# Up projection on TensorE: the low parts of the last 64 inputs, for gate and value side by side on half of the rows each

## The chip, the core and the metric

The kernel runs on one core of a Trainium2 chip. A core has a matrix engine (TensorE, PE in the profile; its weight loads are a row of their own, PEld), a vector engine (VectorE, DVE), a scalar engine (ScalarE, ACT), a general engine (GpSimd, POOL) and a queue engine (SyncE, SP) that issues the DMAs here. The metric is the device time of one execution in microseconds (us).

## The reference

What is computed is an mLSTM recurrence over 16 heads of 768 steps and then two gated feed-forward layers on all 1536 tokens. The up projection, on which the change works, is `x @ w_gate` and `x @ w_val`:

```python
def _moe_ref(x, w_gate, w_val, w_out):       # x (1536, 320), w_gate and w_val (320, 1536), w_out (1536, 320)
    gate = 1.0 / (1.0 + np.exp(-(x @ w_gate)))
    val = x @ w_val
    return (gate * val @ w_out).astype(np.float32)

def _moe2_ref(x, w_gate, w_val, w_out, rms_g):
    rms = np.sqrt(np.mean(x * x, axis=-1, keepdims=True) + 1e-06)
    xn = x / rms * rms_g
    g = xn @ w_gate
    silu = g * (1.0 / (1.0 + np.exp(-g)))
    val = xn @ w_val
    return (silu * val @ w_out).astype(np.float32)
```

The output of the mLSTM goes through `_moe_ref` (layer 0 below) and then `_moe2_ref` (layer 1).

## The kernel before, in words

TensorE multiplies in a type of 32 bits that keeps fewer bits than float32 (F32R). To come close to float32, each operand is held as a high part and a low part (`x_hi`, `x_lo`; `wgv_hi`, `wgv_lo` for the weights of gate and value; `wo_hi`, `wo_lo` and `h_hi`, `h_lo` for the down projection), and a product is the sum of three: high by high, high by low, low by high.

The 320 inputs of a layer are cut into 128 + 128 + 64. The 64 of the last slot (index 2) stand twice, in rows 0 to 63 and in rows 64 to 127, of `x_hi` and `x_lo`; in the weights the upper 64 rows are replaced by the low part (`split_gv`, L375). So one pass over 128 rows gives high by high and low by high of these 64 at once.

`hidden` (L869) computes one tile of 128 of the 1536 hidden features, number f = 0 to 11, for gate (m = 0) and value (m = 1), each in its own PSUM bank. A product for gate is 8 passes, each of which is one weight load and one MATMUL instruction: three (L896, L897, L899) for each of the two full slots, two (L896, L897) for the last. Gate and value together are 16 passes. The banks alternate between two pairs (0 and 1, 2 and 3), so that tile f waits until VectorE has read the banks of tile f - 2 (`hf_done`).

Layer 0 has `NB0` = 6 blocks k of 256 tokens, layer 1 `NB1` = 4 blocks of 384 tokens; each block is 12 calls of `hidden`, and then `project` (L902), the down projection, 3 passes for each f and each 128 tokens (L914, L915, L916). In layer 0 the order in TensorE's program is written by hand: the table `WEAVE` says which pieces of the mLSTM follow after which slot. Piece S is the product of queries and keys (L803): 8 products for each of 12 tiles n, in pairs of heads, one on rows 0 to 39 and one on rows 64 to 103 of the array, each pair into two banks; the profile shows two MATMULs for each product. After S of an even n (slot 2 of a block, in the first block slot 3) `hidden` follows directly; after S of an odd n (slot 6, in the first block 7) the transposes of piece T (L761) come. Pieces N (L822, L830), K (L840) and D (L780, L782) use 120 or 128 rows.

The epilogue of a tile is: ScalarE sigmoid of the gate bank (L527), VectorE product with the value bank into `hf` (L717; in layer 1 also L715), ScalarE `h_hi` (L537), VectorE `h_lo` (L722). In layer 1 the results of `project` stand in banks 0, 1 and 2, which `hidden` uses too, so both functions wait for each other's readers (`hf_done`, `oe_done`).

Of the kernel before, what the change touches and what calls it, by code (L numbers as in the profile page):

```python
# [4 lines left out]
F32 = mybir.dt.float32  # L5
# [5 lines left out]
B, H, S, D = 2, 8, 768, 40  # L11
DM = H * D
FF = 1536
P = 128
NJ = S // P
NT = B * NJ
# [7 lines left out]
NF = FF // P  # L24
# [10 lines left out]
T1 = 3  # L35
# [40 lines left out]
def mlstm_moe_kernel(nc, gates, qk_t, q_t, vok, w_gv, w_o, rms_g, out):  # L76
    ctx = ExitStack()

    def sem(name):
        return ctx.enter_context(nc.semaphore(name))  # L80

    with ctx:
        def sb(name, shape, dt):
            return ctx.enter_context(nc.sbuf_tensor(name, shape, dt))
# [18 lines left out]
        x_hi = sb("x_hi", [P, NT, 3, P], F32R)  # L103
        x_lo = sb("x_lo", [P, NT, 3, P], F32R)
        h_hi = sb("h_hi", [P, NF * N1], F32R)
        h_lo = sb("h_lo", [P, NF * N1], F32R)
        wgv_hi = sb("wgv_hi", [P, GVC, 3, CW], F32R)
# [47 lines left out]
        bank = [ctx.enter_context(nc.psum_tensor(f"bank{i}", [P, 512], F32)) for i in range(8)]  # L155
# [18 lines left out]
        def raw_of(lay, c):  # L174
            ring = (raw0, raw1)[lay]
            r = ring[c % len(ring)]
            if c < GVC:
                return r.rearrange("p (k c) -> p k c", k=3)
            return r[:, 0:FC * DM].rearrange("p (k c) -> p k c", k=FC)
# [5 lines left out]
            return bank[2 * ((n // NF + f) % 2 if lay == 0 else f % 2) + 1]  # L185

        def o_bank(lay, m):
            return bank[2 * (m // B % 2) + m % B] if lay == 0 else bank[m]

        def y_slot(n):  # L190
            return 1 if n == 1 else 0
# [44 lines left out]
        hf_done = sem("hf_done")  # L236
# [5 lines left out]
        yo_done = sem("yo_done")  # L242
        oe_done = sem("oe_done")
        whi0 = sem("whi0")
        wlo0 = sem("wlo0")
        split0 = sem("split0")
        whi1 = sem("whi1")
        wlo1 = sem("wlo1")
        split1 = sem("split1")
# [95 lines left out]
        def _(pool):  # L345
# [22 lines left out]
            def split_gv(lay, c):  # L368
                whi, wlo, split = ((whi0, wlo0, split0), (whi1, wlo1, split1))[lay]
                r = raw_of(lay, c)  # L370
                pool.wait_ge(whi, c + 1)
                pool.tensor_tensor(wgv_lo[:, c, :, :], r[:, 0:2, :], wgv_hi[:, c, 0:2, :].bitcast(F32),  # L372
                                   ALU.subtract).then_inc(wlo, 1)
                pool.wait_ge(wlo, c + 1)
                pool.tensor_tensor(wgv_hi[64:P, c, 2, :], r[64:P, 2, :], wgv_hi[64:P, c, 2, :].bitcast(F32),  # L375
                                   ALU.subtract).then_inc(split, 1)
                pool.wait_ge(split, c + 1)

# [7 lines left out]
            def split(lay, c):  # L386
                if c < GVC:
                    split_gv(lay, c)
                else:
                    split_o(lay, c)  # L390
# [32 lines left out]
            for g in range(NG):  # L423
                nh = min(GH, H - GH * g)
                cs = slice(g * GH * D1, (g * GH + nh) * D1)
# [36 lines left out]
        def _(act):  # L462
# [76 lines left out]
            for k in range(NB0):  # L539
                for slot in range(NF + 4):  # L540
                    if slot < NF:
                        sigmoid(0, NF * k + slot, slot)
                        h_high(0, NF * k + slot, slot)
                    for what in WEAVE[k][slot]:
                        piece(what)
                    if k == 0:
                        for c in SPLIT_AT.get(slot, []):
                            high(0, c)
                    if k == NB0 - 1 and slot < NF and slot % FC == FC - 1:
                        high(1, 2 * (slot // FC))  # L550
                        high(1, 2 * (slot // FC) + 1)
                    if slot >= NF and slot % 2:
                        m = B * k + (slot - NF) // 2
                        act.wait_ge(o_done, m + 1)
                        if m >= B:
                            act.wait_ge(ot_done, m - B + 1)
                        act.activation(y_tok[:, 1 + m % B, 0:DM], o_bank(0, m)[:, 0:DM], ACT.Square,
                                       scale=float(DM) ** -0.5, accum_out=meansq_in[:, m % B:m % B + 1]).then_inc(ss_done, 1)
# [199 lines left out]
        def _(pe):  # L758
# [93 lines left out]
                        pe.wait_ge(r_exp, 2)  # L852
                    turn(bank[7], 1 + n % B).then_inc(ot_done, 1)

            def hidden(lay, k, f, halves=(0, 1)):
                c, i = f // FC, f % FC
                w = (N0, N1)[lay]
                n = NF * k + f if lay == 0 else F1 + NF * k + f
                if lay == 0:
                    if f == 0:  # L860
                        pe.wait_ge(x_done, B * k + B)
                        if k:
                            pe.wait_ge(hf_done, n)
                        else:

                            pe.wait_ge(x_done, B)
                    elif f == 1 and k:
                        pe.wait_ge(yo_done, B * k)
                    elif f >= 2:  # L869
                        pe.wait_ge(hf_done, n - 1)  # L870
                    if k == 0 and i == 0:
                        pe.wait_ge(split0, 2 * (c + 1))
                    xs = slice(B * k, B * k + B)
                else:
                    if f == 0 and 0 in halves:
                        pe.wait_ge(x2_done, T1 * (k + 1))
                        pe.wait_ge(hf_done, n)
                    if k == 0:
                        if f == 1:
                            pe.wait_ge(yo_done, NT)  # L880
                    elif f == 0:
                        pe.wait_ge(oe_done, T1 * (k - 1) + halves[-1] + 1)
                    elif f == 1 and 0 in halves:
                        pe.wait_ge(oe_done, T1 * k)
                    if f >= 2:
                        pe.wait_ge(hf_done, n - 1)
                    if k == 0 and i == 0:
                        pe.wait_ge(split1, 2 * (c + 1))
                    xs = slice(T1 * k, T1 * k + T1)
                cs = slice(i * P, (i + 1) * P)  # L890
                for m in halves:
                    ps, done = ((g_bank, g_done), (v_bank, v_done))[m]
                    ps = ps(lay, n, f)[:, 0:w]
                    wc = 2 * c + m
                    for s in range(3):
                        pe.matmul(ps, wgv_hi[:, wc, s, cs], x_hi[:, xs, s, :], start=(s == 0), stop=False)  # L896
                        mm = pe.matmul(ps, wgv_hi[:, wc, s, cs], x_lo[:, xs, s, :], start=False, stop=(s == 2))  # L897
                        if s < 2:
                            pe.matmul(ps, wgv_lo[:, wc, s, cs], x_hi[:, xs, s, :], start=False, stop=False)  # L899
                    mm.then_inc(done, 1)  # L900

            def project(lay, k, t, half):  # L902
                n0 = NF * k if lay == 0 else F1 + NF * k
                h = (h0, h1)[lay]
                if half == 0:
                    pe.wait_ge(hf_done, n0 + (NF - 1 if lay == 0 or t < 2 else NF))
                ts = slice(t * P, (t + 1) * P)
                ps = o_bank(lay, B * k + t if lay == 0 else t)[:, 0:DM]
                for f in range(half * NF // 2, (half + 1) * NF // 2):
                    if t == 0:  # L910
                        pe.wait_ge(h_done, n0 + f + 1)
                        if k == 0 and f % FC == 0:
                            pe.wait_ge((split0, split1)[lay], GVC + f // FC + 1)
                    pe.matmul(ps, h[0][:, f, ts], wo_hi[:, f, :], start=(f == 0), stop=False)  # L914
                    pe.matmul(ps, h[0][:, f, ts], wo_lo[:, f, :], start=False, stop=False)  # L915
                    mm = pe.matmul(ps, h[1][:, f, ts], wo_hi[:, f, :], start=False, stop=(f == NF - 1))  # L916
                if half == 1:
                    mm.then_inc(o_done, 1)
# [11 lines left out]
                        piece(what)  # L930
            for k in range(NB1):
                for f in range(NF):
                    if k and f == 0:
                        hidden(1, k, 0, (0,))
                        hidden(1, k, 0, (1,))
                    elif k and f == 1:
                        hidden(1, k, 1, (1,))
                        hidden(1, k, 1, (0,))
                    else:
                        hidden(1, k, f)  # L940
                    if k == 0 and f in (1, 3):
                        piece(("O", NT - B + f // 2))
                for t in range(T1):
                    for half in range(2):
                        project(1, k, t, half)
# [66 lines left out]
```

## Time and profile before

| | |
|---|---|
| time, median of 3 runs | 526.01 us (525.93 to 529.76) |
| the profiled execution: its own time | 525.22 us |
| its span in the trace | 523.5 us |
| PE busy | 483.7 us (92%), 3417 MATMULs in the trace |
| DVE, ACT, POOL busy | 250.0, 193.8, 123.2 us |
| up projection: L896, L897, L899 | 720 + 720 + 480 MATMULs |
| granted TensorE clock, mean of the span | 0.970 of full speed |

Times are us from the start of the span unless marked ns. A MATMUL's record begins when it begins to read and its length is modelled, so consecutive records overlap (0.28 us long, 0.12 us apart): the distance between starts is what a pass costs. In the groups of section 5 of the page and in the waits, the arrow names what an engine waited for.

### The profile page before, as it was taken

Reading aid. Unit: us, or ns where it says so; the run is one execution under the profiler, and the core shown is the slowest. Engines: PE = TensorE matmul, PEld = TensorE weight load, DVE = VectorE, ACT = ScalarE, POOL = GpSimd, SP = SyncE. Lnnn points to the kernel's source line nnn. Section 1 sums busy time; section 2 is a strip of 40 time slices with the busy share of each in tenths; the row PEclk is TensorE's granted clock in tenths of the full one; section 3 lists DMA queues with packets and bytes.
Section 4 is the critical chain, followed back from the end, with each engine's and each line's share of the span. In section 5 each row is a group of like instructions: output and inputs, shape, how many; then the busy total and the mean of one; then the engine's idle time right before and its main releaser. Section 6 shows DMA issues by size and latency. Waiting matters only on the chain.

```text
span 523.5 us, 8507 instructions
## 1 busy us (share of the span) xinstructions
PE 483.7 (92%) x3417; PEld 469.5 (90%) x3417; DVE 250.0 (48%) x517; ACT 193.8 (37%) x390; POOL 123.2 (24%) x125
## 2 busy tenths in 40 slices
PE   3659885989998999899899999999999999999997
PEld 2658884979997999899899989999999999999997
DVE  6664996165435724561561552762155135604540
ACT  4347532544265325524441574431133123303320
POOL 3749654211411411141001488500000000000000
PEclk9677987999999999999999999999999999999999
DMA  7435360021102201210112142000000000000001
GB/s 256 153 104 156 105 205 2 1 64 57 41 25 61 74 1 30 63 39 1 52 63 114 45 159 85 0 1 14 25 2 1 26 14 0 1 26 13 1 1 38
DMA packets 11148, 27.74 MB, mean 53 GB/s; under 512 B 1366, under 2 KB 5510, under 8 KB 11110
## 3 DMA queue, kind: packets, MB, share of 16 engines
q1 hardware_dynamic: 11110, 27.20, 16.1%
q8 instruction: 27, 0.44, 0.3%
q14 instruction: 11, 0.09, 0.1%
HBM read 25.23 MB, written 1.97 MB: 52 GB/s over the span
## 4 chain that ended last, share of the span: by engine, by line
PE 75%; DVE 11%; ACT 6%; issue 4%; POOL 3%; DVEq 0%; ACTq 0%; POOLq 0%
PE bank L896 16%; PE bank L897 16%; PE bank L899 10%; PE bank L914 8%; PE bank L916 8%; PE bank L915 8%; PE bank L830 3%; DVE hf L717 2%; DVE h_lo L722 1%; PE bank L822 1%; ACT tail L485 1%; ACT L485 1%; PE bank L803 1%; ACT L527 1%; POOL wgv_lo L372 1%
## 5 line engine op out<-in xcount | busy, mean ns | idle before, releaser
L896 PE MATMUL bank<-x_hi,wgv_hi 128*128 128x256 f32 (+1 forms) x720 | 221.0, 312 | 6.2 <-DVE hf L717 3.4
L897 PE MATMUL bank<-x_lo,wgv_hi 128*128 128x256 f32 (+1 forms) x720 | 217.0, 306 | 0.0
L899 PE MATMUL bank<-x_hi,wgv_lo 128*128 128x256 f32 (+1 forms) x480 | 147.2, 307 | 0.0
L896 PEld LDWEIGHTS bank<-x_hi,wgv_hi 128*128 128x128 f32 x720 | 138.9, 193 | 8.5 <-DVE hf L717 4.1
L897 PEld LDWEIGHTS bank<-x_lo,wgv_hi 128*128 128x128 f32 x720 | 139.0, 193 | 0.4
L537 ACT ACTIVATE h_hi<-hf 128x256 fp32r<-128x256 f32 (+1 forms) x120 | 55.3, 461 | 170.1 <-DVE hf L717 170.1
L914 PE MATMUL bank<-wo_hi,h_hi 128*128 128x320 f32 x288 | 90.5, 314 | 5.6 <-DVE h_lo L722 4.2
L899 PEld LDWEIGHTS bank<-x_hi,wgv_lo 128*128 128x128 f32 x480 | 92.6, 193 | 0.0
L915 PE MATMUL bank<-wo_lo,h_hi 128*128 128x320 f32 x288 | 89.9, 312 | 0.0
L916 PE MATMUL bank<-wo_hi,h_lo 128*128 128x320 f32 x288 | 89.9, 312 | 0.0
L717 DVE TENSOR_TENSOR hf<-sg,bank 128x256 f32<-128x256 f32 (+1 forms) x120 | 56.6, 472 | 68.5 <-ACT sg L527 45.7
L722 DVE TENSOR_TENSOR h_lo<-hf,h_hi 128x256 fp32r<-128x256 f32 (+1 forms) x120 | 76.2, 637 | 0.6
L715 DVE TENSOR_TENSOR sg<-sg,bank 128x384 f32<-128x384 f32 x48 | 26.6, 554 | 101.1 <-PE bank L897 91.5
L527 ACT ACTIVATE sg<-bank 128x256 f32<-128x256 f32 (+1 forms) x120 | 50.0, 417 | 38.5 <-PE bank L897 38.1
L914 PEld LDWEIGHTS bank<-wo_hi,h_hi 128*128 128x128 f32 x288 | 54.9, 191 | 6.5 <-DVE h_lo L722 4.4
L915 PEld LDWEIGHTS bank<-wo_lo,h_hi 128*128 128x128 f32 x288 | 54.9, 191 | 0.0
L916 PEld LDWEIGHTS bank<-wo_hi,h_lo 128*128 128x128 f32 x288 | 54.9, 191 | 0.0
L742 DVE SCALAR_TENSOR_TENSOR y_tok<-bank,rstd,g_row 128x320 f32<-128x320 f32 x12 | 6.6, 551 | 55.7 <-POOL rstd L443 55.7
L780 PE MATMUL bank<-causal,ident_b 128*128 128x512 bf16 x24 | 10.6, 442 | 19.2 <-DVE d_rhs L621 8.5
L571 ACT ACTIVATE y_tok<-bank 128x320 f32<-128x320 f32 x12 | 5.3, 438 | 52.8 <-PE bank L916 52.8
L780 PEld LDWEIGHTS bank<-causal,ident_b 128*128 128x128 bf16 x24 | 2.5, 105 | 24.6 <-issue 10.5
L830 PE MATMUL bank<-step,tail 128*128 128x41 f32 x192 | 23.2, 282 | 0.7 <-DVE tail L637 0.6
(106 smaller groups left out, 449.0 us busy)
## 6 DMA issues: line engine op xcount, KB each, us to landing
step<-in_w_gv SPq DMA_DIRECT2D x7, 576.0 KB, 3.9
step<-in_vok SPq DMA_DIRECT2D x12, 324.0 KB, 3.2
step<-in_qk_t SPq DMA_DIRECT2D x24, 160.0 KB
raw_x<-in_w_gv SPq DMA_DIRECT2D x5, 576.0 KB, 4.0
raw_p<-in_w_gv SPq DMA_DIRECT2D x4, 576.0 KB, 5.4
y<-y_tok SPq DMA_DIRECT2D x12, 160.0 KB, 1.8
step<-in_vok SPq DMA_DIRECT2D x10, 180.0 KB, 3.7
step<-in_q_t SPq DMA_DIRECT2D x10, 180.0 KB, 2.5
```

The lines of the kernel that those rows point to most:

```text
L527: act.activation(sg[:, f % 2, 0:w], g_bank(lay, n, f)[:, 0:w], ACT.Sigmoid).then_inc(sg_done, 1)
L537: act.activation(h[0][:, f, :], hf[:, f % 2, 0:w], ACT.Copy).then_inc(hhi_done, 1)
L715: dve.tensor_tensor(sg[:, u, 0:w], sg[:, u, 0:w], g_bank(lay, n, f)[:, 0:w], ALU.mult).then_inc(silu_done, 1)
L717: dve.tensor_tensor(hf[:, u, 0:w], sg[:, u, 0:w], v_bank(lay, n, f)[:, 0:w], ALU.mult).then_inc(hf_done, 1)
L722: dve.tensor_tensor(h[1][:, f, :], hf[:, f % 2, 0:w], h[0][:, f, :].bitcast(F32), ALU.subtract).then_inc(h_done, 1)
L830: mm = pe.matmul(bank[base(n) + 2][:, h * D1:(h + 1) * D1], wexp[b][:, i, c, :], va[b][:, h * D1:(h + 1) * D1], start=True, stop=True)
L896: pe.matmul(ps, wgv_hi[:, wc, s, cs], x_hi[:, xs, s, :], start=(s == 0), stop=False)
L897: mm = pe.matmul(ps, wgv_hi[:, wc, s, cs], x_lo[:, xs, s, :], start=False, stop=(s == 2))
L899: pe.matmul(ps, wgv_lo[:, wc, s, cs], x_hi[:, xs, s, :], start=False, stop=False)
L914: pe.matmul(ps, h[0][:, f, ts], wo_hi[:, f, :], start=(f == 0), stop=False)
L915: pe.matmul(ps, h[0][:, f, ts], wo_lo[:, f, :], start=False, stop=False)
L916: mm = pe.matmul(ps, h[1][:, f, ts], wo_hi[:, f, :], start=False, stop=(f == NF - 1))
```

## The change

In `hidden`, the two products of the last slot's low input part (`x_lo`, slot 2) now go over 64 rows only, where they take the high part of the weights alone: gate on rows 0 to 63, value on rows 64 to 127, one right behind the other, ahead of all other passes of the tile. The low by low term, which the 128-row pass held, is gone. For this the split of the weights is mirrored for value: chunk c odd keeps its high part in rows 64 to 127 and has the low part in rows 0 to 63. The other 14 passes stay as they were, in another order within a slot. So a tile has 16 MATMULs as before, 14 over 128 rows and 2 over 64.

In layer 1, `project` writes banks 4, 5 and 6 in place of 0, 1 and 2; `hidden` no longer waits for `oe_done`, `project` waits for it in place of `hf_done`, and the first two tiles of a block are no longer split or turned round.

```diff
         def o_bank(lay, m):
-            return bank[2 * (m // B % 2) + m % B] if lay == 0 else bank[m]
+            return bank[2 * (m // B % 2) + m % B] if lay == 0 else bank[4 + m]
...
-                pool.tensor_tensor(wgv_hi[64:P, c, 2, :], r[64:P, 2, :], wgv_hi[64:P, c, 2, :].bitcast(F32),
+                ls = slice(0, 64) if c % 2 else slice(64, P)
+                pool.tensor_tensor(wgv_hi[ls, c, 2, :], r[ls, 2, :], wgv_hi[ls, c, 2, :].bitcast(F32),
                                    ALU.subtract).then_inc(split, 1)
...
-            def hidden(lay, k, f, halves=(0, 1)):
+            def hidden(lay, k, f):
...
+                if f >= 2 or lay == 1:
+                    pe.wait_ge(hf_done, n - 1 if f else n)
+                if k == 0 and i == 0:
+                    pe.wait_ge((split0, split1)[lay], 2 * (c + 1))
                 cs = slice(i * P, (i + 1) * P)
-                for m in halves:
+                for m in range(2):
+                    rs = slice(64 * m, 64 * m + 64)
+                    pe.matmul((g_bank, v_bank)[m](lay, n, f)[:, 0:w], wgv_hi[rs, 2 * c + m, 2, cs], x_lo[rs, xs, 2, :],
+                              start=True, stop=False)
+                for m in range(2):
                     ps, done = ((g_bank, g_done), (v_bank, v_done))[m]
                     ps = ps(lay, n, f)[:, 0:w]
                     wc = 2 * c + m
                     for s in range(3):
-                        pe.matmul(ps, wgv_hi[:, wc, s, cs], x_hi[:, xs, s, :], start=(s == 0), stop=False)
-                        mm = pe.matmul(ps, wgv_hi[:, wc, s, cs], x_lo[:, xs, s, :], start=False, stop=(s == 2))
+                        mm = pe.matmul(ps, wgv_hi[:, wc, s, cs], x_hi[:, xs, s, :], start=False, stop=(s == 2))
                         if s < 2:
+                            pe.matmul(ps, wgv_hi[:, wc, s, cs], x_lo[:, xs, s, :], start=False, stop=False)
                             pe.matmul(ps, wgv_lo[:, wc, s, cs], x_hi[:, xs, s, :], start=False, stop=False)
                     mm.then_inc(done, 1)
...
                 if half == 0:
-                    pe.wait_ge(hf_done, n0 + (NF - 1 if lay == 0 or t < 2 else NF))
+                    if lay == 0:
+                        pe.wait_ge(hf_done, n0 + NF - 1)
+                    elif k:
+                        pe.wait_ge(oe_done, T1 * (k - 1) + t + 1)
```

TensorE's program at piece S of block 1 of layer 0, slot 2, between the last passes of tile f = 2 and the first of f = 3, before:

```order
L896 MATMUL bank<-x_hi,wgv_hi 128x256
L897 MATMUL bank<-x_lo,wgv_hi 128x256
L803 MATMUL bank<-step 128x128 [waits e_done,qk_in0]
L803 MATMUL bank<-step 128x128 x7
L896 MATMUL bank<-x_hi,wgv_hi 128x256 [waits hf_done]
L897 MATMUL bank<-x_lo,wgv_hi 128x256
L899 MATMUL bank<-x_hi,wgv_lo 128x256
```

The same place in the changed program:

```order
L896 MATMUL bank<-x_hi,wgv_lo 128x256
L893 MATMUL bank<-x_hi,wgv_hi 128x256
L805 MATMUL bank<-step 128x128 [waits e_done,qk_in0]
L805 MATMUL bank<-step 128x128 x7
L886 MATMUL bank<-x_lo,wgv_hi 128x256 [waits hf_done]
L886 MATMUL bank<-x_lo,wgv_hi 128x256
L893 MATMUL bank<-x_hi,wgv_hi 128x256
```

The two L886 are the passes over 64 rows. They stand at the head of the tile and carry its wait; here they follow on piece S (L805, L803 before), which also works on parts of the rows.

TensorE's program in the last block of layer 1, at the border of two tiles, before:

```order
L896 MATMUL bank<-x_hi,wgv_hi 128x384
L897 MATMUL bank<-x_lo,wgv_hi 128x384
L896 MATMUL bank<-x_hi,wgv_hi 128x384 [waits hf_done]
L897 MATMUL bank<-x_lo,wgv_hi 128x384
L899 MATMUL bank<-x_hi,wgv_lo 128x384
```

The same border in the changed program:

```order
L893 MATMUL bank<-x_hi,wgv_hi 128x384
L886 MATMUL bank<-x_lo,wgv_hi 128x384 [waits hf_done]
L886 MATMUL bank<-x_lo,wgv_hi 128x384
L893 MATMUL bank<-x_hi,wgv_hi 128x384
L895 MATMUL bank<-x_lo,wgv_hi 128x384
L896 MATMUL bank<-x_hi,wgv_lo 128x384
```

Here both neighbours of the 64-row pair are passes over 128 rows. The programs of the other engines and of the queue keep their order.

## Rows read from the trace of the kernel before

**Rows 1.** The page, sections 1, 2 and 5: busy times, clock, and one group of VectorE.

```profile
PE 483.7 (92%) x3417; PEld 469.5 (90%) x3417; DVE 250.0 (48%) x517; ACT 193.8 (37%) x390; POOL 123.2 (24%) x125
...
PEclk9677987999999999999999999999999999999999
...
L715 DVE TENSOR_TENSOR sg<-sg,bank 128x384 f32<-128x384 f32 x48 | 26.6, 554 | 101.1 <-PE bank L897 91.5
```

**Rows 2.** Busy time by stretch: end of block 0, blocks 1 to 5, layer 1.

```profile
53.00:88.00 35.00, 25.73 (x188) 23.93 (x187) 33.78 (x51) 13.99 (x24) 20.32 (x13) 0.93 0.35 109
97.00:311.00 214.00, 204.72 (x1663) 198.00 (x1663) 102.23 (x243) 94.83 (x200) 47.07 (x52) 1.00 0.16 52
311.00:523.50 212.50, 209.41 (x1291) 208.96 (x1289) 82.97 (x155) 57.95 (x123) 20.32 (x15) 1.00 0.05 18
```

**Rows 3.** Waits of PE from 0 to 97 us: total, times, longest.

```profile
PE bank L780 <- POOL d_rhs L400: 5.3, 1, 5.3
PE bank L914 <- DVE h_lo L722: 4.2, 1, 4.2
...
PE bank L896 <- DVE hf L717: 2.3, 1, 2.3
```

**Rows 4.** Waits of PE from 97 us to the end.

```profile
PE bank L780 <- issue: 4.4, 3, 1.5
PE bank L822 <- DVE x_lo L691: 2.0, 4, 0.7
PE bank L803 <- ACT tail L485: 1.4, 1, 1.4
PE bank L896 <- DVE hf L717: 1.1, 1, 1.1
PE bank L896 <- DVE y_tok L743: 0.4, 1, 0.4
```

**Rows 5.** Timeline of PE's matmuls, 149.8 to 153 us: start, length, instruction, count.

```profile
149.78 0.28 PE L897 MATMUL bank<-x_lo,wgv_hi 128*128 128x256 f32 x1
...
151.45 0.28 PE L897 MATMUL bank<-x_lo,wgv_hi 128*128 128x256 f32 x1
151.66 1.16 PE L803 MATMUL bank<-step 40*128 40x128 f32 x16
152.75 0.39 PE L896 MATMUL bank<-x_hi,wgv_hi 128*128 128x256 f32 x1
152.98 0.28 PE L897 MATMUL bank<-x_lo,wgv_hi 128*128 128x256 f32 x1
```

**Rows 6.** Timeline of the weight loads (PEld) in the same stretch.

```profile
151.34 0.19 PEld L897 LDWEIGHTS bank<-x_lo,wgv_hi 128*128 128x128 f32 x1
151.66 0.97 PEld L803 LDWEIGHTS bank<-step 40*128 40x128 f32 x16
152.75 0.19 PEld L896 LDWEIGHTS bank<-x_hi,wgv_hi 128*128 128x128 f32 x1
```

**Rows 7.** Line L803 from 151.2 to 153 us: shortest, median, longest ns.

```profile
L803 PE MATMUL bank<-step x16: 272/272/373, 151.7 to 152.6; 40*128 40x128 f32 x16
```

**Rows 8.** The chain of waits, 147 to 150 us: start, length, what.

```profile
149.07 1.09 ACT tail L485 x2
```

**Rows 9.** Timeline of PE around 124.8 us.

```profile
124.73 0.28 PE L897 MATMUL bank<-x_lo,wgv_hi 128*128 128x256 f32 x1
124.85 0.79 PE L822 MATMUL bank<-cst,step 120*128 120x123 f32 x6
```

**Rows 10.** Timeline of PE around 131.8 us.

```profile
131.65 0.28 PE L897 MATMUL bank<-x_lo,wgv_hi 128*128 128x256 f32 x1
131.77 0.49 PE L761 MATMUL bank<-ident,y_tok 128*128 128x128 f32 x3
```

**Rows 11.** Timeline of PE, 119.3 to 120.7 us.

```profile
119.33 0.28 PE L897 MATMUL bank<-x_lo,wgv_hi 128*128 128x256 f32 x1
119.54 1.16 PE L803 MATMUL bank<-step 40*128 40x128 f32 x16
120.64 0.55 PE L761 MATMUL bank<-ident,y_tok 128*128 128x128 f32 x3
```

**Rows 12.** Timeline of PE in layer 1, around 473 us.

```profile
472.00 0.33 PE L899 MATMUL bank<-x_hi,wgv_lo 128*128 128x384 f32 x1
...
473.91 0.33 PE L896 MATMUL bank<-x_hi,wgv_hi 128*128 128x384 f32 x1
```

More of the change, by code:

```diff
@@ L868, in hidden @@
                         pe.wait_ge(yo_done, B * k)
[L869 to L872, printed above, removed]
                     xs = slice(B * k, B * k + B)
                 else:
-                    if f == 0 and 0 in halves:
+                    if f == 0:
                         pe.wait_ge(x2_done, T1 * (k + 1))
[L877 to L888, printed above, removed]
+                    elif f == 1 and k == 0:
+                        pe.wait_ge(yo_done, NT)
                     xs = slice(T1 * k, T1 * k + T1)
+                if f >= 2 or lay == 1:
+                    pe.wait_ge(hf_done, n - 1 if f else n)
+                if k == 0 and i == 0:
+                    pe.wait_ge((split0, split1)[lay], 2 * (c + 1))
                 cs = slice(i * P, (i + 1) * P)
-                for m in halves:
+                for m in range(2):
[3 more added lines that the diff above has]
+                for m in range(2):
                     ps, done = ((g_bank, g_done), (v_bank, v_done))[m]
@@ L932, in _ @@
                 for f in range(NF):
[L933 to L940, printed above, removed]
+                    hidden(1, k, f)
                     if k == 0 and f in (1, 3):
```

## The prediction

> **What bounds the kernel now.** I read the page first: PE is busy 92% of the span, no other engine above 48%, and the granted clock is at full speed but for the first quarter [rows 1]. Then the busy times by stretch [rows 2]: in blocks 1 to 5 of layer 0 (97 to 311 us) PE is busy 204.7 of 214 us, in layer 1 209.4 of 212.5; only the end of block 0 is different, where VectorE is busy 33.8 of 35 us and PE 25.7. The waits say the same: after 97 us PE waits 9.3 us in all, in waits of at most 1.5 us [rows 4], before it there are waits of 5.3, 4.2 and 2.3 us for GpSimd and VectorE [rows 3]. In layer 1 VectorE waits for PE, 91.5 us on one line [rows 1]. So from 97 us on, what TensorE's stream of passes gains or loses is the time, nearly one to one. In block 0 most of it is hidden.
>
> What a pass costs is read from the distance of starts. Layer 0: 14 passes from 149.78 to 151.45, 0.119 us each [rows 5]. Layer 1: 11 passes from 472.00 to 473.91, 0.174 us each [rows 12]. A weight load takes 0.19 us by its record, but in the stream it begins while earlier passes run and costs nothing [rows 6].
>
> **What a pass over part of the rows costs.** The kernel has such passes already: piece S puts two products side by side, on rows 0 to 39 and 64 to 103. Two things are to be seen.
>
> First, they do run together. The 16 records of S last 1.16 us, 0.27 of it the last record's own length and 0.10 a longer first record (373 against 272 ns), so the other 15 steps take 0.79 us of streaming, 0.112 us for two of them (8 pairs, 7 steps between them) [rows 5, 7]. The transposes, 128 columns of float32 like S, but on all rows, take (0.49 - 0.27) / 2 = 0.11 us each [rows 10]. A pair costs what one costs.
>
> Second, going into and out of them is dear. The last pass of 128 rows before S starts at 151.45. The next weight load should begin before that pass is through, but it begins at 151.66, 0.21 us later, and the first product's record is 0.10 us longer than its like, since its load was not done ahead [rows 5 to 7]. So streaming begins 0.31 us after the last pass in place of 0.119: entering costs **0.19 us**. On the way out the last S record starts at 151.66 + 1.16 - 0.27 = 152.55, the next weight load at 152.75, and the first L896 has 0.39 in place of 0.28 us; streaming begins 0.31 us after, where the 128 columns need 0.11: leaving costs **0.19 to 0.20 us**. It is no late semaphore: what S waits for, ScalarE's exponentials, ended at 150.16 [rows 8], and pieces that start with a wait of their own but use 120 or 128 rows, in float32 too, follow at 0.12 us [rows 9, 10]. The next S at 119.54 shows the same 0.21, and its exit into transposes 0.20 us [rows 11]. The array first empties, and then loads weights in the open, whenever the rows in use change from whole to part or back.
>
> **The change part by part.** Removed: 2 of 16 passes over 128 rows. Added: a pair over 64 rows that runs as one, with an entry and an exit, in each of 72 + 48 calls of `hidden`. As the emptying came after 128 columns and after 256 with the same 0.19, I take it as not depending on columns; the two passes of the pair start some ns apart.
>
> - Layer 0: before 16 x 0.119 = 1.904. After: 14 + 1 passes, 15 x 0.119 = 1.785, + 0.19 + 0.19 = 2.165. Cost 0.26 us a tile.
> - Layer 1: one pass less, -0.174, + 0.38: cost 0.21 us a tile.
>
> Sum over what is on the path: blocks 1 to 5, 60 x 0.26 = 15.6; layer 1, 48 x 0.21 = 10.1 (PE has no gap there that could take it up: the 3 us that the stretch is short of busy time are the end and one start [rows 2, 4]). To be taken off:
>
> - S of an even tile is followed directly by `hidden`, whose pair uses part of the rows too, so S's exit and the pair's entry both go: 4 times in blocks 1 to 5, 4 x 0.38 = 1.5.
> - Waits of PE that the longer tile in front shortens, each by at most 0.26: 4 of L822 for `x_lo`, one of L803, one for `hf`, one for `y_tok` [rows 4]: 7 x 0.26 = 1.8. The 4.4 us before L780 stay: they follow on PE's own piece K and move with it.
>
> Block 0: 12 x 0.26 = 3.1 if all of it is on the path, 0 if none, since PE waits there 11.8 us in three waits [rows 3] and VectorE holds its end [rows 2]; with the lower clock a switch may cost more. Nearer to none; I take 1.0. Sum: 15.6 + 10.1 - 1.5 - 1.8 + 1.0 = **+23.4 us**.
>
> The rest I cost at nothing. The wait for `hf_done` now stands before value's bank is written 8 passes earlier, but it is the same count that gate waited for before, and VectorE has done it a tile ahead. The gate bank is complete after a pair, an exit and 7 passes instead of 8, some 0.3 us later in the tile; sigmoid has the 7 passes of value (0.8 us) as cover, and without it VectorE would still have the whole next tile. Moving `project` to banks 4 to 6 takes away waits that never ended last: no `oe_done` reader stands in the waits [rows 4]. GpSimd's mirrored half of the split has the same shape. DMAs are untouched.
>
> The sum against the execution that was profiled: 525.2 + 23.4 = 548.6. The median of the runs is 0.8 us above it, which gives **549 us**.
>
> Of the pages, the Trainium skill's "TensorEngine Tiling (Array Packing)", Key Properties, says that changing the tiling mode, not just the tile, drains the engine, and gives no price. An estimate from "TensorE: Matmul & The Clock Gate" (its phase DRAIN, about 128 cycles, and its section LDWEIGHTS, columns divided by 1.2 GHz) would be 0.053 + 0.107 = 0.16 us a change in place of the 0.19 read here, and the sum would be 60 x 0.20 + 48 x 0.146 - 1.3 - 1.4 + 0.8 = +17, 542 us. The row decides: it holds the whole of it in this very stream.
>
> **Rivals.**
>
> - **Faster: the change of rows costs nothing.** If S pays for something of its own (40 rows, or the float32 type), the pair is one pass and its loads are done ahead: 60 x 0.119 + 48 x 0.174 = 15.4 us less, 525.2 - 15.4 = 510 us. For it: rows of S are all there is, never a 64-row pass in F32R. Against: the entry of 120-row float32 pieces costs nothing [rows 9], so type and odd row counts are excluded, and the exit goes into plain 128-row passes and costs the same. It decides for faster below 0.06 us a change. Chance 0.08. The Trainium skill's page "TensorE: Matmul & The Clock Gate", Packing small matmuls, speaks for it: loads for another row group are pulled ahead, and a packed pair spans one matmul and about 4 ns. By that rule it would be these 510 us; the records of S agree within the pairs and not at their borders.
> - **Only one of the two borders costs**, as the pair's first load could be pulled ahead: 60 x 0.07 + 48 x 0.02 - 1 = +4, 529 us; or the 64-row passes run as whole ones, no pairs and no switches, and the change does not do what it says: 16 passes, 525 us. Against both: the symmetric 0.19 and 0.20, and the pairs of S. Chance 0.05.
> - **The borders cost, and the halves don't overlap**, since 256 or 384 columns of two operands could be read at half speed: another 0.119 or 0.174 a tile, 549 + 15.4 = 564 us. Against: the pairs at 0.112 us [rows 5, 7]. Chance 0.04.
> - **The clock falls** because PE stands idle 0.4 of each 2.2 us. In the trace it fell around the long waits of the first quarter, and stayed at full speed in all of blocks 1 to 5, where PE waits often [rows 1, 2]. At 0.93, as at the end of block 0 [rows 2], the 430 us after it would be 30 us longer: 580 us. Chance 0.03.
>
> **How the numbers follow.** The forecast has 0.80. Its own range: +-0.03 us on 216 borders is 6.5 us, block 0 from -1 to +2, the covered waits from 0 to 3: 540 to 558. The cases outside it hold 0.2; widened a little for what I have not seen, 538 to 560. Faster by over 1% (below 520.7, about what a measurement of this kernel can tell): the first rival, 0.08. Within 1%: the second, 0.05. Slower: the rest, 0.87.
>
> **What would show it.** Right: starts of the two L886 some ns apart; 0.2 us from the last 128-row pass to the pair's first load in layer 0 (0.26 in layer 1, as its stream is 0.05 longer), and 0.2 us (0.26) from the pair to the next load; first records 0.1 us longer; tiles of 2.17 us in layer 0 and 2.99 in layer 1; a busy share of PE that falls while no wait for another engine grows. The place behind an S in slot 2 has no gap. Wrong: L886 at the stream's distance from both neighbours (first rival), 0.119 us apart (third), or a granted clock below 1.00 after 97 us (fourth).

## The result: 544.0 us, 3.4% slower

| | before | changed |
|---|---|---|
| time, median | 525.97 us (525.62 to 529.76, 4 runs) | 544.02 us (543.63 to 547.02, 4 runs) |
| ratio, 95% interval | | 1.0343 (1.0291 to 1.0396) |
| profiled execution: time, span | 525.22, 523.5 us | 543.63, 541.9 us |

The span is 18.4 us longer; the sum had 23.4. From the page of the changed kernel, the lines that answer to [rows 1]:

```profile
PE 507.2 (94%) x3417; PEld 454.8 (84%) x3417; DVE 247.2 (46%) x517; ACT 199.6 (37%) x390; POOL 122.9 (23%) x125
...
L886 PEld LDWEIGHTS bank<-x_lo,wgv_hi 64*128 64x128 f32 x240 | 22.6, 185 | 27.3 <-issue 19.6
```

PE's busy share rose, against what I had said it would do. A half pass's record is 0.37 to 0.44 us long in the timelines below and starts together with its own weight load, so the records fill the gap at a border. The better witness is PEld: 84% in place of 90, and 27.3 us without a load ahead of L886, most of it with no engine to blame ("issue"). A part of the fall is only that the two loads of a pair lie side by side and count once.

The timeline of PE in layer 1, and of its weight loads at the same place:

```profile
440.81 0.34 PE L893 MATMUL bank<-x_hi,wgv_hi 128*128 128x384 f32 x1
441.08 0.44 PE L886 MATMUL bank<-x_lo,wgv_hi 64*128 64x384 f32 x2
441.45 0.44 PE L893 MATMUL bank<-x_hi,wgv_hi 128*128 128x384 f32 x1
441.73 0.34 PE L895 MATMUL bank<-x_lo,wgv_hi 128*128 128x384 f32 x1
```

```profile
440.64 0.19 PEld L893 LDWEIGHTS bank<-x_hi,wgv_hi 128*128 128x128 f32 x1
441.08 0.18 PEld L886 LDWEIGHTS bank<-x_lo,wgv_hi 64*128 64x128 f32 x2 [0.25 <-issue]
441.45 0.19 PEld L893 LDWEIGHTS bank<-x_hi,wgv_hi 128*128 128x128 f32 x1 [0.18 <-issue]
```

The two half passes together take 0.44 us, as long as one: they run side by side. The loads of the pair and of the pass behind it start 0.27 and 0.37 us after the start of the pass ahead of them, where in the stream a load starts together with that pass, and the first record at each border is 0.10 us longer. From the last whole pass (440.81) to the second of the next tile (441.73) it is 0.92 us; the pair's own stream and two steps of 0.17 are 0.52 of it. The rest, 0.40 us, is the price of one visit to partial rows (going in and coming out), and the visit saves one pass of 0.17.

The same between two tiles of layer 0:

```profile
123.48 0.28 PE L893 MATMUL bank<-x_hi,wgv_hi 128*128 128x256 f32 x1
123.69 0.39 PE L886 MATMUL bank<-x_lo,wgv_hi 64*128 64x256 f32 x2
124.01 0.39 PE L893 MATMUL bank<-x_hi,wgv_hi 128*128 128x256 f32 x1
124.23 0.28 PE L895 MATMUL bank<-x_lo,wgv_hi 128*128 128x256 f32 x1
```

From 123.48 to 124.23 it is 0.75 us, three steps of 0.119 are 0.36 of it, and the visit costs 0.39 us: 0.27 a tile after the pass that it saves, where the sum had 0.26.

Behind piece S (L805) in layer 0 there is no gap, as expected: the pair's record begins while S runs out.

```profile
104.68 1.16 PE L805 MATMUL bank<-step 40*128 40x128 f32 x16
105.59 0.37 PE L886 MATMUL bank<-x_lo,wgv_hi 64*128 64x256 f32 x2
```

**Where the time went.** The first pass of a block's `project` (L914) is a mark that both kernels have. In the timeline of the kernel before, in block 0, block 5, and blocks 0 and 3 of layer 1:

```profile
76.21 0.42 PE L914 MATMUL bank<-wo_hi,h_hi 128*128 128x320 f32 x1
312.30 0.31 PE L914 MATMUL bank<-wo_hi,h_hi 128*128 128x320 f32 x1
356.99 0.31 PE L914 MATMUL bank<-wo_hi,h_hi 128*128 128x320 f32 x1
504.41 0.31 PE L914 MATMUL bank<-wo_hi,h_hi 128*128 128x320 f32 x1
```

The same four in the changed kernel:

```profile
76.34 0.41 PE L914 MATMUL bank<-wo_hi,h_hi 128*128 128x320 f32 x1 [0.18 <-DVE hf L719]
320.02 0.31 PE L914 MATMUL bank<-wo_hi,h_hi 128*128 128x320 f32 x1
367.30 0.31 PE L914 MATMUL bank<-wo_hi,h_hi 128*128 128x320 f32 x1
522.82 0.31 PE L914 MATMUL bank<-wo_hi,h_hi 128*128 128x320 f32 x1
```

| stretch between marks | tiles | before | changed | more | sum had |
|---|---|---|---|---|---|
| up to the first mark | 12 | 76.21 | 76.34 | 0.1 | 1.0 |
| blocks 1 to 5 | 60 | 236.09 | 243.68 | 7.6 | 12.3 |
| layer 1, block 0 | 12 | 44.69 | 47.28 | 2.6 | 2.5 |
| layer 1, blocks 1 to 3 | 36 | 147.42 | 155.52 | 8.1 | 7.6 |

Layer 1 came a little dearer than forecast (0.223 us a tile for 0.21). Blocks 1 to 5 came 4.7 us cheaper, although a tile's passes there cost what the sum had. The waits of PE from 97 us on say where it went; [rows 4] had five lines, 9.3 us, and here only two are left, 4.7 us:

```profile
PE bank L782 <- issue: 3.8, 3, 1.3
PE bank L805 <- ACT tail L487: 0.9, 1, 0.9
```

### The profile page after: what moved, and what is told of

Read it like the earlier page. It is cut to its first block, busy times and chain, and to the rows that moved or that the text cites. A ratio compares the mean times of both kernels' runs of the same rounds, so it can differ in the third digit from the quotient of the medians.

```text
span 541.9 us, 8508 instructions
## 1 busy us (share of the span) xinstructions
PE 507.2 (94%) x3417; PEld 454.8 (84%) x3417; DVE 247.2 (46%) x517; ACT 199.6 (37%) x390; POOL 122.9 (23%) x125
## 4 chain that ended last, share of the span: by engine, by line
PE 85%; DVE 8%; POOL 3%; issue 2%; ACT 1%; DVEq 0%; POOLq 0%; ACTq 0%
PE bank L893 22%; PE bank L896 12%; PE bank L895 12%; PE bank L914 8%; PE bank L915 8%; PE bank L916 8%; PE bank L886 7%; PE bank L832 3%; PE bank L805 2%; PE bank L763 1%; DVE h_lo L724 1%; PE bank L824 1%; POOL wgv_lo L372 1%; PE bank L782 1%; PE bank L842 1%
## 5 line engine op out<-in xcount | busy, mean ns | idle before, releaser
L893 PE MATMUL bank<-x_hi,wgv_hi 128*128 128x256 f32 (+1 forms) x720 | 213.0, 323 | 0.0
L893 PEld LDWEIGHTS bank<-x_hi,wgv_hi 128*128 128x128 f32 x720 | 131.7, 191 | 18.3 <-issue 9.3
L895 PE MATMUL bank<-x_lo,wgv_hi 128*128 128x256 f32 (+1 forms) x480 | 146.6, 305 | 0.0
L914 PE MATMUL bank<-wo_hi,h_hi 128*128 128x320 f32 x288 | 90.5, 314 | 5.7 <-DVE h_lo L724 4.2
L895 PEld LDWEIGHTS bank<-x_lo,wgv_hi 128*128 128x128 f32 x480 | 92.0, 192 | 0.0
L916 PE MATMUL bank<-wo_hi,h_lo 128*128 128x320 f32 x288 | 89.8, 312 | 0.0
L724 DVE TENSOR_TENSOR h_lo<-hf,h_hi 128x256 fp32r<-128x256 f32 (+1 forms) x120 | 72.4, 605 | 0.6
L914 PEld LDWEIGHTS bank<-wo_hi,h_hi 128*128 128x128 f32 x288 | 54.8, 190 | 6.9 <-DVE h_lo L724 4.4
L916 PEld LDWEIGHTS bank<-wo_hi,h_lo 128*128 128x128 f32 x288 | 54.9, 191 | 0.0
L886 PE MATMUL bank<-x_lo,wgv_hi 64*128 64x256 f32 (+1 forms) x240 | 49.2, 406 | 4.3 <-POOL wgv_hi L377 2.6
L886 PEld LDWEIGHTS bank<-x_lo,wgv_hi 64*128 64x128 f32 x240 | 22.6, 185 | 27.3 <-issue 19.6
```

Source lines behind the costliest of these rows:

```text
L724: dve.tensor_tensor(h[1][:, f, :], hf[:, f % 2, 0:w], h[0][:, f, :].bitcast(F32), ALU.subtract).then_inc(h_done, 1)
L886: pe.matmul((g_bank, v_bank)[m](lay, n, f)[:, 0:w], wgv_hi[rs, 2 * c + m, 2, cs], x_lo[rs, xs, 2, :], start=True, stop=False)
L893: mm = pe.matmul(ps, wgv_hi[:, wc, s, cs], x_hi[:, xs, s, :], start=False, stop=(s == 2))
```

## The experiments

From here on a stage's time is the distance between two such marks in the run's timeline. That matters, because the start of the program scatters: the first up projection began between 23.6 and 27.3 us in the profiled runs, in programs that up to there differ at most in the rows that the split of the weights writes and in the tile's first two passes, and single times carry that scatter: 23.6 in the kernel before and in the changed one, 25.9 with both halves on the same rows, 27.3 and 23.9 in the last two kernels, which begin alike.

### Undo the half rows alone

```diff
-                    rs = slice(64 * m, 64 * m + 64)
+                    rs = slice(0, P)
```

> The changed kernel, but the two low passes at the head of each tile run over all 128 rows (the low part of the weights multiplies the low part of the inputs too, as before the change). Order of passes, waits and banks of the change stay. Theory (the border between whole and partial rows costs 0.19 to 0.20 us each way): 16 whole passes and no border, 525 to 527 us, the weight loads follow the stream, no gap at a tile's head. Rival (the new order, the wait at the head or the banks cost): 540 us or more, gaps stay.

Measured: 526.91 us (10 runs), ratio to the kernel before 1.0013 (0.9983 to 1.0044). The marks:

```profile
78.61 0.41 PE L914 MATMUL bank<-wo_hi,h_hi 128*128 128x320 f32 x1
314.70 0.31 PE L914 MATMUL bank<-wo_hi,h_hi 128*128 128x320 f32 x1
359.39 0.31 PE L914 MATMUL bank<-wo_hi,h_hi 128*128 128x320 f32 x1
506.81 0.31 PE L914 MATMUL bank<-wo_hi,h_hi 128*128 128x320 f32 x1
```

236.09, 44.69 and 147.42 us: each stage takes what it took before, to 0.01 us. So the new order, the place of the wait and banks 4 to 6 cost nothing and bring nothing; the whole loss is in the partial rows.

### Both halves on the same rows

```diff
-                    rs = slice(64 * m, 64 * m + 64)
+                    rs = slice(0, 64)
```

> The changed kernel, but value's half pass runs on rows 0 to 63 like gate's (value takes the wrong part of the weights there, so its low term is wrong). Same number of rows, same borders, only not side by side. Theory (the pair of the change runs as one pass): one pass more in each tile, 0.12 us in layer 0 and 0.17 in layer 1, 544 + 7 + 8 = about 559 us, and the second half pass starts a stream distance behind the first in place of 4 ns. Rival (the pair was serial all along, its start times only look equal): 544 us.

Measured: 561.58 us in one run, span 559.8, with a start 2.3 us later than that of the changed kernel. The timeline in layer 1:

```profile
451.20 0.34 PE L893 MATMUL bank<-x_hi,wgv_hi 128*128 128x384 f32 x1
451.47 0.62 PE L886 MATMUL bank<-x_lo,wgv_hi 64*128 64x384 f32 x2
452.01 0.44 PE L893 MATMUL bank<-x_hi,wgv_hi 128*128 128x384 f32 x1
```

The two records now cover 0.62 us, 0.18 more than side by side, and the next load comes at 0.54 after the first in place of 0.37. So the pair of the change does save its pass. The entry is as it was (0.27).

### Two visits to partial rows in a tile

```diff
-                for m in range(2):
-                    rs = slice(64 * m, 64 * m + 64)
-                    pe.matmul((g_bank, v_bank)[m](lay, n, f)[:, 0:w], ..., start=True, stop=False)
                 for m in range(2):
...
+                    rs = slice(64 * m, 64 * m + 64)
+                    pe.matmul(ps, wgv_hi[rs, wc, 2, cs], x_lo[rs, xs, 2, :], start=True, stop=False)
                     for s in range(3):
```

> The changed kernel, but value's half pass stands at the head of value's passes, behind gate's seven, so each tile goes into partial rows and out again twice. Theory: for each tile one more entry and exit and one more pass: 0.38 + 0.12 = 0.50 us in layer 0, 0.40 + 0.17 = 0.57 in layer 1: 544 + 72 x 0.50 + 48 x 0.57 = 607 us if nothing is covered, about 603 with block 0 covered. Rival (the cost is one of starting a tile, not of each border): 544 + 15 = 559 us.

Measured: 602.27 us in one run, span 600.5. The last two marks (its line L912):

```profile
404.69 0.31 PE L912 MATMUL bank<-wo_hi,h_hi 128*128 128x320 f32 x1
581.43 0.31 PE L912 MATMUL bank<-wo_hi,h_hi 128*128 128x320 f32 x1
```

176.74 - 155.52 = 21.2 us for 36 tiles, 0.59 a tile where 0.57 were expected. The price is paid at each border.

### No half passes

The two half passes are left out, with the high by low term of the last 64 inputs; 14 passes stay.

```diff
-                for m in range(2):
-                    rs = slice(64 * m, 64 * m + 64)
-                    pe.matmul((g_bank, v_bank)[m](lay, n, f)[:, 0:w], ..., start=True, stop=False)
...
-                        mm = pe.matmul(ps, ..., x_hi[:, xs, s, :], start=False, stop=(s == 2))
+                        mm = pe.matmul(ps, ..., x_hi[:, xs, s, :], start=(s == 0), stop=(s == 2))
```

> The changed kernel without the two half passes (high weights by low inputs of the last 64 are left out): 14 whole passes. Theory: against 16 passes 2 x 0.119 x 60 = 14 us and 2 x 0.174 x 48 = 17 us less, but the waits of PE on ScalarE and VectorE in layer 0 come back or grow by some us: 526 - 31 + 5 = about 500 us; so the pair with its borders costs some 44 us in the changed kernel, where the bare pass is 15. Rival (the half passes are cheap and the loss is elsewhere): 530 us or more.

Measured: 503.31 us in one run. The pair costs 40.7 us in the changed kernel, though its bare pass is 15. In blocks 1 to 3 of layer 1, where PE waits for nobody, the marks stand at 347.57 and 482.51 us: 134.94 for 155.52, 0.57 us a tile, which is the visit of 0.40 and the pass of 0.17. And PE's waits from 97 us on grew to 16.0 us; of five lines the two that grew most:

```profile
PE bank L824 <- DVE x_lo L693: 5.4, 4, 1.4
...
PE bank L889 <- DVE hf L719: 4.0, 9, 1.3
```

The longest wait for `x_lo` is 0.7 us with 16 passes a tile, 1.4 with 14, and there is none in the changed kernel: it is what is left of another engine's time after PE's.

### A known load in layer 0, with no border

To the kernel before, one or two whole passes more in each tile of layer 0 (terms are counted twice in the result). The diff is that with one; with two, the condition on `m` is not there.

```diff
                         mm = pe.matmul(ps, wgv_hi[:, wc, s, cs], x_lo[:, xs, s, :], start=False, stop=(s == 2))
+                        if lay == 0 and s == 1 and m == 0:
+                            pe.matmul(ps, wgv_hi[:, wc, s, cs], x_lo[:, xs, s, :], start=False, stop=False)
```

> The same with one more whole pass, of gate alone: 0.12 us a tile, 7.1 us in blocks 1 to 5. Theory (a wait takes up what all tiles since the last meeting of the engines added, 4 to 5 tiles x 0.12, up to its own length): 3 to 4 us covered, 526 + 3.5 = 529.5 us. Rival (a wait takes up what the one tile ahead of it added): 0.12 x 7 = 0.8 covered, 532.3 us.

> The kernel before, with two more whole passes in each tile of layer 0 (a low pass of gate and one of value doubled, so the result takes those terms twice): 0.24 us more a tile, with no border, about what the change adds to a tile there. Theory (the missing part of the expected loss went into waits of PE that were covered whole, N 0.5 to 0.8 us each, and those of block 5): 60 x 0.24 = 14.3 us less 6 covered, 526 + 8 = 534 us, and the waits for x_lo and hf are gone from the profile. Rival (the borders are cheaper in layer 0 than read, and waits cover only what one tile adds, 1.8 us): 526 + 12.5 = 538.5 us.

Measured: 529.18 and 534.90 us, one run each. The marks of blocks 0 and 5 with one pass more, and then with two (line L916 in both):

```profile
77.09 0.39 PE L916 MATMUL bank<-wo_hi,h_hi 128*128 128x320 f32 x1
316.25 0.31 PE L916 MATMUL bank<-wo_hi,h_hi 128*128 128x320 f32 x1
```

```profile
77.56 0.41 PE L916 MATMUL bank<-wo_hi,h_hi 128*128 128x320 f32 x1 [0.19 <-DVE hf L717]
322.00 0.31 PE L916 MATMUL bank<-wo_hi,h_hi 128*128 128x320 f32 x1
```

| added in blocks 1 to 5 | of it seen | covered |
|---|---|---|
| one pass: 60 x 0.119 = 7.1 us | 239.16 - 236.09 = 3.1 | 4.0 |
| two passes: 14.3 us | 244.44 - 236.09 = 8.4 | 5.9 |
| the change: 15.6 - 1.5 = 14.1 us | 7.6 | 6.5 |

Of the first 7 us more than half are covered, of the next 7 only 1.9. So the missing loss of the change is nothing about borders: a load of this size without any border loses some 6 us there too. With two passes the lines for `x_lo`, `hf` and `y_tok` are gone from the waits, and 4.5 us are left.

### Fewer borders for the same half passes

If the border is the cost, several pairs should share one. From the kernel before, with value's rows mirrored as in the change, and only in blocks 1 to 3 of layer 1: the half passes of four tiles stand in a row at the end of the first of them, behind its 14 whole passes. For that the eight banks are a ring of four tiles. A second kernel does it with groups of two (`f % 2` and `range(2)` in the lines below, the same ring).

```diff
+            if n >= F1 + NF:
+                return bank[2 * (f % 4)]
...
+                first = f % 4 == 0
...
+                if first:
+                    pe.wait_ge(hf_done, n)
+                    if f == 0:
+                        pe.wait_ge(oe_done, T1 * k)
+                    for j in range(4):
+                        cj, ij = (f + j) // FC, (f + j) % FC
+                        for m in range(2):
+                            rs = slice(64 * m, 64 * m + 64)
+                            mm = pe.matmul((g_bank, v_bank)[m](1, n + j, f + j)[:, 0:N1],
+                                           wgv_hi[rs, 2 * cj + m, 2, ij * P:(ij + 1) * P], x_lo[rs, xs, 2, :],
+                                           start=(j > 0), stop=(j == 0))
```

> The kernel before, changed in blocks 1 to 3 of layer 1 alone: the half passes of four tiles stand together, four pairs in a row at the end of the first of the four, with all eight banks as a ring of four tiles. So 36 tiles save a pass, and 9 groups pay for one entry and one exit. Theory (cost goes by borders, not by half passes): -36 x 0.1735 + 9 x 0.40 = -2.7 us, 523.3 us, ratio 0.995. Rival (each pair costs by itself what it does in the change, 0.23 us a tile): +8 us, 534 us.

> The kernel with groups in blocks 1 to 3 of layer 1, but groups of two tiles: 18 groups instead of 9, the same number of half passes. Theory (cost by borders): -36 x 0.1735 + 18 x 0.40 = +0.95 us against the kernel before in these three blocks, so 3.6 us more than groups of four; groups of one (the change) have +8.1 there. Rival (the gain of the groups comes from the ring of eight banks, not from fewer borders): -2.6 us as with four.

Measured, in fours: 525.00 us (12 runs), ratio 0.9952 (0.9922 to 0.9982), a gain that is clear of the noise and far below 2%. The medians, 526.35 and 525.00, differ by less than the 2.7 us expected and carry the scatter of the starts; the stages below do not. The timeline at a group (eight half passes, L939), and the last two marks around it:

```profile
361.69 0.31 PE L957 MATMUL bank<-wo_hi,h_hi 128*128 128x320 f32 x1
...
379.81 0.34 PE L924 MATMUL bank<-x_hi,wgv_hi 128*128 128x384 f32 x1
380.07 0.96 PE L939 MATMUL bank<-x_lo,wgv_hi 64*128 64x384 f32 x8
380.97 0.44 PE L924 MATMUL bank<-x_hi,wgv_hi 128*128 128x384 f32 x1
...
506.53 0.31 PE L957 MATMUL bank<-wo_hi,h_hi 128*128 128x320 f32 x1
```

One gap of 0.26 in front, one exit, and eight products in 0.96 us. In twos, one run, 529.14 us with a late start (26.3 us):

```profile
359.74 0.31 PE L957 MATMUL bank<-wo_hi,h_hi 128*128 128x320 f32 x1
508.29 0.31 PE L957 MATMUL bank<-wo_hi,h_hi 128*128 128x320 f32 x1
```

| blocks 1 to 3 of layer 1 | visits to partial rows | stage | against before | a visit |
|---|---|---|---|---|
| the change | 36 | 155.52 us | +8.1 | (8.1 + 6.25) / 36 = 0.40 us |
| in twos | 18 | 148.55 | +1.1 | 0.41 |
| in fours | 9 | 144.84 | -2.6 | 0.41 |

6.25 us is 36 x 0.1735, the whole passes saved, the same in all three. The cost is linear in the visits, and the ring of eight banks, which both grouped kernels have, brings nothing by itself.

### The groups in block 0 of layer 1 too

Tiles 4 to 11 of that block also go in fours. Their pairs write bank 7, from which VectorE and ScalarE read the last transposes of layer 0's output (piece O, after tile 3), so a wait for `x2_done` is needed. First I put it at the head of tile 4:

```diff
-            if n >= F1 + NF:
+            if n >= F1 + 4:
...
+                if k == 0 and f == 4:
+                    pe.wait_ge(x2_done, NT)
+                    pe.wait_ge(split1, GVC)
```

> The kernel with groups of four in blocks 1 to 3 of layer 1, and now also tiles 4 to 11 of block 0. Theory: 8 tiles save a pass, 2 groups pay: -8 x 0.1735 + 2 x 0.40 = -0.6 us more, 526.0 - 3.2 = 522.8 us, ratio to the kernel before 0.994. Rival (the groups' saving is used up by the later gate of the first tile): no further gain, 523.4 us or more.

Measured: 526.66 us (12 runs), ratio 1.0005 (0.9981 to 1.0029): a miss, nothing is left of the gain. Blocks 1 to 3 take 144.84 us as in the first version in fours, but block 0 of layer 1 takes 48.2 us (marks at 316.66 and 364.86) in place of 44.69. The timeline at tile 4, and the busy times by stretch behind it (the column behind POOL's is the granted clock):

```profile
338.80 0.49 PE L766 MATMUL bank<-ident,y_tok 128*128 128x128 f32 x3
341.78 0.69 PE L927 MATMUL bank<-x_hi,wgv_hi 128*128 128x384 f32 x1 [2.49 <-DVE x_lo L696]
342.26 0.52 PE L930 MATMUL bank<-x_lo,wgv_hi 128*128 128x384 f32 x1
342.58 0.52 PE L931 MATMUL bank<-x_hi,wgv_lo 128*128 128x384 f32 x1
```

```profile
341.80:345.00 3.20, 3.20 (x11) 3.20 (x12) 0.00 (x0) 0.00 (x0) 0.00 (x0) 0.54 0.00 0
```

The transposes had only just been issued, and the chain through ScalarE and VectorE behind them takes 2.5 us. PE stood still for it, and then ran for about 3 us at the lower clock level, 1.2 GHz (a granted clock of 0.54 over the stretch), with passes 0.32 us apart in place of 0.17. The wait of 2.5 us and some ten passes of 0.15 us more each account, roughly, for the 3.5 us lost. So the wait was moved 14 passes down, to the pairs that need it:

```diff
-                    pe.wait_ge(x2_done, NT)
...
                 if first:
                     pe.wait_ge(hf_done, n)
+                    pe.wait_ge(x2_done, NT)
```

> As the kernel with groups of four in tiles 4 to 11 of block 0 of layer 1 too, but the wait for the last x_lo stands before the four pairs (which write bank 7, where the transposes of that x_lo are read) and no longer at the head of tile 4, 14 passes = 2.4 us earlier. Theory (all that was lost there is this wait of 2.5 us behind the transposes and the 3.4 us of lower clock that it brought): PE no longer waits there, up to the projection of block 0 it takes 44.7 - 0.6 = 44.1 us, and blocks 1 to 3 keep 144.8: 526.2 - 3.2 = 523 us, ratio 0.994. Rival (the groups don't suit block 0): 48 us up to that projection again.

Measured: 522.81 us (9 runs) against 527.51 of the kernel before on the same chip, ratio 0.9924 (0.9887 to 0.9960). Its marks of block 5 and of block 0 of layer 1:

```profile
312.85 0.31 PE L960 MATMUL bank<-wo_hi,h_hi 128*128 128x320 f32 x1
...
357.17 0.31 PE L960 MATMUL bank<-wo_hi,h_hi 128*128 128x320 f32 x1
```

44.32 us for 44.69 before, -0.4 where -0.6 was expected, and blocks 1 to 3 take 144.84 again. By stages it is 2.6 + 0.4 = 3.0 us faster than the kernel before. The ratio shows some 4 us; the rest is in no stage of the profiled executions, and is taken to be scatter at the start, which no run separates. This version beats both kernels, the kernel before by under 1%.

## Why the prediction was right, and which term was off

**Direction and mechanism: right.** The step that carried it was reading piece S's borders: a visit to partial rows costs 0.19 us in and 0.19 to 0.20 out, in 128-column float32 products of 40 rows. In F32R passes of 64 rows and 384 columns it is 0.27 + 0.10 - 0.17 = 0.20 in, and 0.40 for the whole visit; with 256 columns it is 0.39. That the cost doesn't depend on columns held.

**The pair saves its pass: right**, shown by both halves on the same rows.

**What was costed at nothing: right.** The whole-row version has the stages of the kernel before to 0.01 us. One sign was read wrongly: the busy share of PE was to fall, and it rose from 92 to 94%.

**Layer 1, 10.1 us: measured 10.7.** A visit there is 0.40 us, not 0.38.

**The mis-sized term: "waits of PE that the longer tile in front shortens, each by at most 0.26", 1.8 us.** The known loads show 4.0 us covered of 7.1 and 5.9 of 14.3, the change 6.5 of 14.1. I let a wait take up only what the tile right in front of it had gained; that rule would have covered 0.8 us of the 7.1. What fits is that the engine that PE waits for does not move with PE: its work starts at a common point, and all that PE got to do since then comes out of the wait. One such wait was followed through. ScalarE's timeline, before and then changed, over the tiles ahead of the wait for `x_lo` in block 1:

```profile
97.44 1.28 ACT L527 ACT_TABLE_LOAD   x1
...
108.76 0.47 ACT L507 ACTIVATE x_hi<-bank 128x384 fp32r<-128x384 f32 x1
```

```profile
97.53 1.28 ACT L529 ACT_TABLE_LOAD   x1
...
108.84 0.47 ACT L509 ACTIVATE x_hi<-bank 128x384 fp32r<-128x384 f32 x1
```

Three table loads of 1.28 us each (the first is shown) stand in this stretch, and between them steps of ScalarE and VectorE that wait for each other; 11 us of it are shifted by 0.08 to 0.09 us only, while PE had four longer tiles to do (the fifth there follows on S). PE came to piece N at 109.97 with a wait before, and at 110.19 without one now. A second thing made the waits look short: their length in the profile counts from the modelled end of the last record, 0.28 us after its start, where a pass costs 0.12. The 0.67 shown at 109.97 was 0.96 from start to start, 0.84 more than the stream's distance. And the 4.4 us before L780, which were to stay, shrank to 3.8.

**Block 0, 1.0 us: measured 0.1.** VectorE was busy 33.9 of the 35 us from 53 to 88 us, as before, which fits that it held this stage; the measured value lies at the lower end of the bound. Some luck may be in it: the granted clock of those 35 us was 0.98 in this execution and 0.93 before [rows 2], and no run separates the two.

**The clock: the rival did not come.** It stayed at full speed from 97 us on with a gap in every tile. In the run with the early wait a standstill of 2.5 us was followed by the lower level, but its length is not the whole story. The kernel before and the groups of four both wait 1.38 us at the same S, and behind it the first stays at full speed [rows 2], while the second ran about 3 us at 1.2 GHz (a granted clock of 0.50):

```profile
264.98 1.16 PE L808 MATMUL bank<-step 40*128 40x128 f32 x16 [1.38 <-ACT tail L490]
```

```profile
267.00:270.00 3.00, 3.00 (x16) 3.00 (x16) 2.16 (x5) 1.43 (x4) 0.00 (x0) 0.50 0.00 0
```

From the mark of block 3 to that of block 4 (232.71 and 280.31) this execution took 47.6 us, the kernel before 46.1. So a wait of 1.4 us can be followed by a drop or not, and what decides stays open.

**The two rules of the Trainium skill.** That a change of tiling mode drains the engine (the Trainium skill, "TensorEngine Tiling (Array Packing)", Key Properties) agrees with every border here. With the estimate of 0.16 us made from the figures of the Trainium skill's "TensorE: Matmul & The Clock Gate" a visit would be 0.32 us, and the trace has 0.39 to 0.40. The rule of the Trainium skill's "TensorE: Matmul & The Clock Gate", Packing small matmuls, that a pair spans one matmul and about 4 ns, holds inside the pair (0.44 us for both in layer 1, and 0.44 for a half pass that stands alone in the version with two visits). It says nothing of borders with passes over all rows.

## What to carry to other kernels

Count visits to partial rows, not products on them: here a visit is 0.40 us, 2.3 whole passes of 384 columns or 3.4 of 256. A visit for one pair, which saves one pass, loses; four pairs in one visit win. When PE is the bound but waits now and then, ask of each wait from which point on the other engine runs by itself; added PE time since that point is covered up to the wait's length from start to start, and time taken from PE comes back as wait in the same way. A new wait goes to the instruction that needs it, not to the head of its tile.

## What the runs showed of the hardware that was not expected

- The price of a visit is nearly the same for 40 rows of float32 with 128 columns (0.38 to 0.39 us) and for 64 rows of F32R with 256 and 384 columns (0.39 and 0.40). The entry into a piece on 120 rows costs nothing [rows 9].
- A standstill of PE of 2.5 us in the midst of a dense stream was followed by about 3 us at 1.2 GHz, and one of 1.4 us in one execution and not in another, while gaps of 0.27 us in every tile of 3 us never were.
- PE's busy share went up (92 to 94%) in a kernel whose array does less; the share of the weight loads fell (90 to 84%).
